# Pooling the first batch's keys on TensorE instead of VectorE, with the opening loads reordered

## The chip, the cores and the metric

The kernel runs on one core of a Trainium2 chip. The metric is the device time of one execution in microseconds; for the kernel before it is 1462.22 us, the median of 3 runs (1461.35 to 1463.22).

## The reference

Attention over pooled keys and values, then two feed-forward blocks, all in float32:

```python
B, H, S, D = 8, 8, 576, 64
k_p = k.reshape(B, H, S // 8, 8, D).mean(axis=3)      # 72 pooled keys per head
v_p = v.reshape(B, H, S // 8, 8, D).mean(axis=3)
attn = softmax(q @ k_p.T / sqrt(D))                   # per head
x = (attn @ v_p), heads side by side                  # 4608 tokens x 512
h = max(x @ w1, x @ w2, x @ w3)                       # 512 -> 768
x2 = h @ w_mid                                        # 768 -> 512
u = x2 @ w_in                                         # 512 -> 2048
out = (u - tanh(u)) @ w_out                           # 2048 -> 512
```

## The kernel before, in words

Every engine walks the same hand-made list `ORDER` (made by `make_order`, L91) and picks the entries that concern it; semaphores do the rest. Tokens are treated in 36 steps of 128 for the attention and in 9 tiles of 512 for the feed-forward blocks; the first tile's first layer is done in two halves of 256 tokens. The products of the feed-forward blocks are made as three passes over a high part and a low part of both operands, so each weight block ("piece") is loaded raw, rounded to its high part by ScalarE (`piece_high`, entry `high`) and has the remainder taken by VectorE or GpSimd (`piece_low`, entry `low`; the pieces named in `LOW_ON_POOL`, from the third weight block on, go to GpSimd). The matmuls of the attention are plain float32, and each of them appears in the profile as two instructions on PE and two weight loads on PEld.

The opening, where the change lies, runs as follows before it.

- SyncE issues all loads from one queue, in program order (L370 to L389): the four head pairs' keys of batch 0 (`k_first`, dims on partitions, 576 tokens x 4 pairs), the first 128 tokens' `q`, then, after a wait for the first keys, the second `q`, batch 0's values (`v_first`, tokens on partitions, 5 blocks of up to 128 tokens), then weight blocks, `q` and later keys and values alternately.
- TensorE multiplies a tile of ones with itself 14 times (`keep_warm`, L565), into a bank that nobody reads. VectorE meanwhile sums batch 0's keys by eights (`reduce_k`, L779), one instruction per pair, into `k_pooled`.
- TensorE makes the scores of steps 0 and 1 (`score`, L487; waits for `q` and for all four sums), pools the values by a product with a 0/1 matrix (`poolers`, `pool_first_v`, L506), does 14 more products of ones, and then `attend(0)` (L527), which waits for both steps' probabilities. VectorE takes row maxima, shifts, normalizes and transposes (L796 to L820); ScalarE does the exponentials (L661) between.
- The result goes through ScalarE (L666) and VectorE (L826) as high and low parts into `x`, and the first layer (`layer1`, L544) starts: blocks m = 0 to 5, each 3 x 12 matmuls into PSUM banks 0 to 3 in turn. ScalarE copies the first of the three banks (L672), VectorE takes the maxima of the other two (L836, L841), ScalarE and VectorE make the high and low part of `h1` (L680, L847). A bank is free for the next block once it is so read.
- After block 0 of the first half come the scores of steps 2 and 3, and in ScalarE's list their exponentials stand ahead of the high part of the fourth weight block, `("high", 3)`. GpSimd takes that block's low part (L468), for which `layer1` of block 3 waits.

```python
    o = [("kred", 0, p) for p in range(PAIRS)] + [
        ("warm", 14), ("score", 0), ("score", 1), ("pool_v",), ("warm", 14), ("norm", 0), ("high", 0), ("norm", 1),
        ("high", 1), ("low", 0), ("attend", 0), ("low", 1), ("high", 2)]
```

Of the kernel before, what the change touches and what calls it, by code (L numbers as in the profile page):

```python
# [5 lines left out]
F32 = mybir.dt.float32  # L6
F32R = mybir.dt.float32r
U8 = mybir.dt.uint8
ALU = mybir.AluOpType
# [3 lines left out]
P = 128  # L13
# [76 lines left out]

def make_order():  # L91

    o = [("kred", 0, p) for p in range(PAIRS)] + [
        ("warm", 14), ("score", 0), ("score", 1), ("pool_v",), ("warm", 14), ("norm", 0), ("high", 0), ("norm", 1),
        ("high", 1), ("low", 0), ("attend", 0), ("low", 1), ("high", 2)]
    waiting = []

    def then(*entries):
        for e in entries:
            o.append(e)  # L100
            if e[0] == "score" and e[1] in LAST_STEP[:-2]:
# [12 lines left out]
    def split(*pieces):  # L114
        return [(part, i) for i in pieces for part in ("high", "low")]

    waiting.extend([[("kred", 1, 0), ("kred", 1, 1)], [("kred", 1, 2), ("kred", 1, 3)],
                    [("vred", 1, 0)], [("vred", 1, 1)], [("vred", 1, 2)]])
    after_l1 = [[("score", 2), ("score", 3), ("high", 3), ("norm", 2)], [("high", 4), ("norm", 3)], [("high", 5)],
                [("high", 6)], [("attend", 1)], [("high", 7)]]  # L120
    for m in range(MC1):
        l1(0, m, 0, HALF)
        then(*after_l1[m])
        if m > 1:
            fill()

    for t in range(NT):
        a = 4 * t + 4
        after_l1 = [[("score", a), ("score", a + 1), ("norm", a)], [("norm", a + 1)], [],
                    [("score", a + 2), ("score", a + 3), ("norm", a + 2)], [("norm", a + 3)], []]  # L130
        after_l2 = [[], [("attend", t + 2)], [], []]
        if t == 0:
            after_l2 = [[], [], [("attend", t + 2)], []]
        if t == 0:
            after_l1[4:] = [[], [("norm", a + 3)]]
        if t == NT - 1:
            after_l1 = [[("load", ("out", 0)), ("load", ("in", 0)), ("load_x2",)],
                        split(8) + [("load", ("out", 1)), ("load", ("in", 1)), ("x2split",)],
                        split(9, 10) + [("load", ("out", 2)), ("load", ("in", 2))],
                        split(11, 12) + [("load", ("in", 3))],  # L140
                        split(13) + [("load", ("in", 4))],
                        split(14) + [("load", ("in", 5))]]
# [27 lines left out]
assert [e[1] for e in ORDER if e[0] == "high"] == list(range(len(PIECES) - len(LATE)))  # L170


def fused_attention_mlps(nc, q, k, v_0, v, w123_in, w_mid, w_in, w_out, out):
    x2_dram = nc.dram_tensor("x2_scratch", (KC1, P, TOKENS), F32, kind="Internal").ap()

    with ExitStack() as ctx:
        def sem(name):
            return ctx.enter_context(nc.semaphore(name))
# [10 lines left out]
        def overlay(*lists):  # L189
# [39 lines left out]
        (_, w_mid_raw, k_first, v_first), (q_t, k_raw, v_raw, k_pooled, v_pooled, probs, row_max, row_sum,  # L229
         row_eps, row_inv, _, w_mid_s, h1, first_copy, best, x2_stage), (w_out_raw,), (  # L230
            w_out_s, u_sq, poly, tanh_h, g, is_big) = overlay(
            front + [("w_mid_raw", mid_shape, F32), ("k_first", [P, PAIRS, KEYS, POOL], F32), ("v_first", [P, 5, DM], F32)],
            attention + [("w_mid_s", mid_shape, F32R), ("h1", h1_shape, F32R)] + work,
            [("w_out_raw", [P, MC2, 2, DM], F32)],
            [("w_out_s", [P, MC2, 2, DM], F32R), ("u_sq", [P, 2, TB], F32),
# [13 lines left out]
        shift_ready = sem("shift_ready")  # L249
        ones_ready = sem("ones_ready")  # L250
        q_in = [sem(f"q_in{n}") for n in range(QSLOTS)]
        k_first_in = [sem(f"k_first_in{n}") for n in range(PAIRS)]
        v_first_in = [sem(f"v_first_in{n}") for n in range(2)]
        poolers_made = sem("poolers_made")
        v_first_summed = sem("v_first_summed")
# [78 lines left out]
        def _(sp):  # L334
# [7 lines left out]
            def load_k(b, p):  # L342
                if b >= B:
                    return
                i = PAIRS * (b - 1) + p
                if i >= 2:
                    sp.wait_ge(k_reduced, PAIRS + i - 1)
                sp.dma_start(k_raw[:, i % 2].rearrange("p n t -> p (n t)"), k[b, p]).then_inc(k_in[i % 2], 16)

            def load_v(b, p):  # L350
                if b >= B:
# [15 lines left out]
                sp.dma_start(x2_raw[(t + 1) % 2][:, 1], x2_dram[:, :, bass.ds(t * TB, TB)].rearrange("c p n -> p c n"))\  # L367
                    .then_inc(x2_in, 16)

            for p in range(PAIRS):  # L370
                sp.dma_start(k_first[:, p].rearrange("p n t -> p (n t)"), k[0, p]).then_inc(k_first_in[p], 16)
            load_q(0)
            sp.wait_ge(k_first_in[0], 16)
            load_q(1)
            sp.dma_start(v_first[:, 0:4], v_0[0:4 * P].rearrange("(u p) f -> p u f", p=P)).then_inc(v_first_in[0], 16)
            sp.dma_start(v_first[0:D, 4], v_0[4 * P:S]).then_inc(v_first_in[1], 16)
            load_piece(0)
            load_q(2)
            load_piece(1)
            load_q(3)  # L380
            load_piece(2)
            for p in range(2):
                load_k(1, p)
            load_piece(3)
            load_piece(4)
            for p in range(2):
                load_v(1, p)
# [84 lines left out]
        def _(pe):  # L472
# [2 lines left out]

            def score(n):
                pe.wait_ge(q_in[n % QSLOTS], 16 * (n // QSLOTS) + 16)
                pe.wait_ge(k_reduced, PAIRS * ((n * P + P - 1) // S) + PAIRS)
                if n >= 2:
                    pe.wait_ge(shifted, n - 1)  # L480
                    wait_x(pe, product_of(n) - 1)
                for g in range(GROUPS):
                    b = (n * P + g * BLK) // S
                    for pr in range(PAIRS):
                        for odd in range(2):
                            half = slice(odd * D, (odd + 1) * D)
                            mm = pe.matmul(scores_of(n)[pr * BLK:(pr + 1) * BLK, odd, g, :],  # L487
                                           q_t[half, n % QSLOTS, pr, g * BLK:(g + 1) * BLK],
                                           k_pooled[half, b % 2, pr, :], start=True, stop=True)
                mm.then_inc(scored, 1)  # L490

            def open_bank(entry, n=0):
# [2 lines left out]
                    pe.wait_ge(drained[bank], before)  # L495
                return bank

            def pool_first_v():

                pe.wait_ge(poolers_made, 3)  # L500
# [67 lines left out]
            for entry in ORDER:  # L568
                if entry[0] == "warm":
                    keep_warm(entry[1])  # L570
                if entry[0] == "pool_v":
                    pool_first_v()
                if entry[0] == "score":
# [73 lines left out]
        def _(act):  # L647
            def piece_high(i):
                act.wait_ge(piece_in[i], 16)
                _, raw, hi, _ = piece(i)  # L650
                nc.scalar.activation(hi, raw, ACT.Copy).then_inc(piece_hi, 1)

            def copy_first_v():
                act.wait_ge(v_first_summed, 1)
                nc.scalar.activation(v_pooled[:, 0].rearrange("p c o d -> p (c o d)"), psum[:, 3, 0:3 * P], ACT.Copy)\
                    .then_inc(v_first_pooled, 1)
# [42 lines left out]
            for entry in ORDER:  # L699
                if entry[0] == "high":  # L700
                    piece_high(entry[1])
                if entry[0] == "pool_v":
                    copy_first_v()
                if entry[0] == "score":
# [62 lines left out]
        @block.vector  # L767
        def _(dve):
            def reduce_k(b, p):
                if b == 0:  # L770
                    dve.wait_ge(k_first_in[p], 16)
                    src = k_first[:, p]
                else:
                    i = PAIRS * (b - 1) + p
                    dve.wait_ge(k_in[i % 2], 16 * (i // 2) + 16)
                    if b >= 2:
                        dve.wait_ge(scored, LAST_STEP[b - 2] + 1)
                    src = k_raw[:, i % 2]
                nc.vector.tensor_reduce(k_pooled[:, b % 2, p, :], src, AX.X, ALU.add).then_inc(k_reduced, 1)  # L779

            def reduce_v(b, p):
                i = 3 * (b - 1) + p
# [192 lines left out]
```

## Time and profile before

| | |
|---|---|
| median of 3 runs | 1462.22 us |
| the profiled execution | 1461.79 us |
| its span | 1459.9 us |
| PE busy | 1448.3 us (99% of the span) |
| PEld busy (weight loads) | 1198.4 us (82%) |
| DVE / ACT / POOL busy | 903.5 / 506.0 / 25.7 us |

The sum of an edit is made against the profiled execution, 1461.79 us; the median of the runs lies 0.43 us above it. PE is busy in all but about 11.6 us of the span. Times in the rows are microseconds from the span's start.

### The profile page before, as it was taken

To read this page: it belongs to the slowest core of one execution; us is meant where nothing else is said; L and a number is where in the kernel's file an instruction comes from. 1 tells how busy PE (TensorE), PEld (TensorE's weight loads), DVE (VectorE), ACT (ScalarE), POOL (GpSimd) and SP (SyncE) were. 2 spreads that over 40 slices of the span, in tenths; PEclk is the share of its full clock that TensorE was granted. 3 is DMA by queue.
4 is the path that set the end of the run, shared out by engine and by line. 5 is a ranking of instruction groups with operands and counts; after the bars stand their busy time and mean duration, and the time that the engine had idled before them with its cause. 6 is when DMAs were issued, how large, how long until landed. Compare 5 with 4: busy or idle time off the path is not lost.

```text
span 1459.9 us, 23041 instructions
## 1 busy us (share of the span) xinstructions
PE 1448.3 (99%) x9480; PEld 1198.4 (82%) x9480; DVE 903.5 (62%) x1461; ACT 506.0 (35%) x889; POOL 25.7 (2%) x28
## 2 busy tenths in 40 slices
PE   8999999999999999999999999999999999999998
PEld 7988888888888878788888888888888888888887
DVE  6856363646464626265766776667677676767666
ACT  3322122212121212144444444434444443444443
POOL 2400000000000000000000000000000000000000
PEclk9999999999999999999999999999999999999999
DMA  9241213130302000243010010100001010000000
GB/s 341 78 134 47 89 46 89 46 91 29 116 19 75 16 30 1 97 139 110 1 38 22 0 59 1 59 0 29 29 0 58 0 46 12 23 35 1 29 1 29
DMA packets 34652, 75.33 MB, mean 52 GB/s; under 512 B 3136, under 2 KB 3136, under 8 KB 34560
## 3 DMA queue, kind: packets, MB, share of 16 engines
q1 hardware_dynamic: 34560, 74.07, 15.5%
q8 instruction: 62, 1.02, 0.3%
q14 instruction: 30, 0.25, 0.1%
HBM read 55.18 MB, written 18.87 MB: 51 GB/s over the span
## 4 chain that ended last, share of the span: by engine, by line
PE 96%; DVE 2%; DMA 1%; ACT 0%; issue 0%; SPq 0%; DVEq 0%; ACTq 0%
PE psum L544 30%; PE psum L610 26%; PE psum L593 26%; PE psum L558 10%; PE psum L527 2%; PE psum L487 2%; DMA v_first<-in_v 1%; PE psum L565 0%; DVE g L884 0%; DVE poly L895 0%; DVE poly L899 0%; DVE psum L901 0%; DMA k_first<-in_k 0%; DVE probs L815 0%; DVE poly L905 0%
## 5 line engine op out<-in xcount | busy, mean ns | idle before, releaser
L544 PE MATMUL psum<-x,w 128*128 128x512 f32 (+1 forms) x2160 | 451.2, 369 | 1.7 <-DVE x L826 1.0
L544 PEld LDWEIGHTS psum<-x,w 128*128 128x128 f32 x2160 | 375.6, 188 | 71.8 <-issue 1.9
L610 PE MATMUL psum<-w_out_s,g 128*128 128x512 f32 x1728 | 415.1, 389 | 0.9 <-DVE g L884 0.9
L610 PEld LDWEIGHTS psum<-w_out_s,g 128*128 128x128 f32 x1728 | 324.3, 188 | 68.9 <-DVE g L884 1.7
L895 DVE SCALAR_TENSOR_TENSOR poly<-poly,u_sq 128x512 f32<-128x512 f32 x144 | 99.7, 692 | 235.7 <-ACT poly L734 235.7
L726 ACT ACTIVATE u_sq<-psum 128x512 f32<-128x512 f32 x144 | 86.2, 599 | 425.8 <-PE psum L593 425.8
L593 PE MATMUL psum<-x_odd,w_in_s 128*128 128x512 f32 x960 | 230.0, 389 | 0.0
L593 PEld LDWEIGHTS psum<-x_odd,w_in_s 128*128 128x128 f32 x960 | 180.2, 188 | 37.4
L593 PE MATMUL psum<-x_even,w_in_s 128*128 128x512 f32 x768 | 184.5, 389 | 0.0
L593 PEld LDWEIGHTS psum<-x_even,w_in_s 128*128 128x128 f32 x768 | 144.2, 188 | 29.9
L558 PE MATMUL psum<-h,w_mid_s 128*128 128x512 f32 x648 | 150.8, 391 | 0.0
L558 PEld LDWEIGHTS psum<-h,w_mid_s 128*128 128x128 f32 x648 | 121.0, 188 | 28.3 <-issue 3.4
L680 ACT ACTIVATE h<-best 128x512 fp32r<-128x512 f32 (+1 forms) x60 | 35.3, 589 | 275.5 <-DVE best L841 275.5
L734 ACT ACTIVATE poly<-u_sq,shift_col 128x512 f32<-128x512 f32 x144 | 104.3, 725 | 2.2 <-DVE g L884 2.2
L905 DVE COPY_PREDICATED poly<-is_big,psum 128x512 f32<-128x512 uint8 x144 | 104.9, 729 | 0.1
L884 DVE TENSOR_TENSOR g<-poly,g 128x512 fp32r<-128x512 f32 x144 | 99.7, 692 | 6.3 <-ACT g L720 1.5
L901 DVE TENSOR_TENSOR psum<-psum,tanh_h 128x512 f32<-128x512 f32 x144 | 99.8, 693 | 0.0
L899 DVE SCALAR_TENSOR_TENSOR poly<-poly,psum 128x512 f32<-128x512 f32 x144 | 98.0, 680 | 0.0
L841 DVE TENSOR_TENSOR best<-psum,best 128x512 f32<-128x512 f32 (+1 forms) x60 | 38.3, 638 | 89.2 <-PE psum L544 87.7
L720 ACT ACTIVATE g<-poly 128x512 fp32r<-128x512 f32 x144 | 90.9, 631 | 5.0 <-DVE poly L905 5.0
L727 ACT ACTIVATE tanh_h<-psum 128x512 f32<-128x512 f32 x144 | 85.5, 594 | 0.0
L836 DVE TENSOR_TENSOR best<-psum,first_copy 128x512 f32<-128x512 f32 (+1 forms) x60 | 37.5, 625 | 77.4 <-PE psum L544 77.4
(53 smaller groups left out, 697.9 us busy)
## 6 DMA issues: line engine op xcount, KB each, us to landing
v_raw<-in_v SPq DMA_DIRECT2D x21, 512.0 KB, 4.3
q_t<-in_q SPq DMA_DIRECT2D x36, 256.0 KB, 3.4
x_scratch<-x_stage SPq DMA_DIRECT2D x36, 256.0 KB, 3.1
out<-out_stage SPq DMA_DIRECT2D x36, 256.0 KB, 2.1
k_raw<-in_k SPq DMA_DIRECT2D x28, 288.0 KB, 2.9
x_raw_odd<-x_scratch SPq DMA_DIRECT2D x5, 1024.0 KB, 5.2
w_raw<-in_w SPq DMA_DIRECT2D x6, 768.0 KB, 13.9
x_raw_even<-x_scratch SPq DMA_DIRECT2D x4, 1024.0 KB, 5.1
```

The lines of the kernel that those rows point to most:

```text
L544: mm = pe.matmul(psum[:, bank, 0:hi - lo], w123[:, m, ws, n, c, :], x[:, xs, c, lo:hi], start=(c == 0 and ws + xs == 0), stop=(c == KC1 - ...
L558: mm = pe.matmul(psum[:, bank, :], w_mid_s[:, ws, m, c * P:(c + 1) * P], h1[:, xs, m, :], start=(m == 0 and ws + xs == 0), stop=(m == MC1 ...
L593: mm = pe.matmul(psum[:, 4 + m % 4, :], w_in_s[:, m, ws, c, :], xs_tile[:, xs, c, :], start=(c == 0 and ws + xs == 0), stop=(c == KC1 - 1 ...
L610: mm = pe.matmul(psum[:, j, :], g[:, m % 4, gs, j * P:(j + 1) * P], w_out_s[:, m, ws, :], start=(m == 0 and gs + ws == 0), stop=(m == MC2 ...
L720: nc.scalar.activation(g[:, m % 4, 0, :], poly[:, m % 2], ACT.Copy).then_inc(g_hi_ready, 1)
L726: nc.scalar.activation(u_sq[:, m % 2], bank, ACT.Square).then_inc(sq_done, 1)
L734: nc.scalar.activation(poly[:, m % 2], u_sq[:, m % 2], ACT.Square, bias=shift_col[:, 0:1])\
L884: nc.vector.tensor_tensor(g[:, m % 4, 1, :], poly[:, m % 2], as_f32(g[:, m % 4, 0, :]), ALU.subtract).then_inc(g_ready, 1)
L895: nc.vector.scalar_tensor_tensor(out=p, in0=p, scalar=OFFSET, in1=u, op0=ALU.add, op1=ALU.mult)\
L899: nc.vector.scalar_tensor_tensor(out=p, in0=p, scalar=C2, in1=bank, op0=ALU.mult, op1=ALU.mult)
L901: nc.vector.tensor_tensor(bank, bank, tanh_h[:, m % 2], ALU.subtract).then_inc(dve_step, 1)
L905: nc.vector.copy_predicated(p, is_big[:, m % 2], bank).then_inc(h_drained, 1)
```

## The change

Batch 0's keys arrive as tokens on partitions (a new input `k_0`, 576 rows of 512 floats) in five loads, four of 128 tokens and one of 64. TensorE pools them: per block of tokens four products, each with 128 dims of the keys as the weights and 16 columns of `poolers` as the moving operand (8 columns for the last block), into bank 1; ScalarE copies the 128 x 288 result into `k_pooled`, and `score(0)` waits for that copy. The products of ones are dealt out between the blocks: 8, 2, 2 and 1 ahead of the scores, 8 before the values' pooling, 10 after it. VectorE's four sums for batch 0 go away. SyncE no longer waits before the second `q`, and the second weight block is loaded ahead of the third `q`, the fourth ahead of batch 1's first keys. `("high", 3)` moves ahead of the scores of steps 2 and 3.

```diff
-    o = [("kred", 0, p) for p in range(PAIRS)] + [
-        ("warm", 14), ("score", 0), ("score", 1), ("pool_v",), ("warm", 14), ("norm", 0), ("high", 0), ("norm", 1),
-        ("high", 1), ("low", 0), ("attend", 0), ("low", 1), ("high", 2)]
+    o = [("warm", 8), ("pool_k", 0), ("warm", 2), ("pool_k", 1), ("warm", 2), ("pool_k", 2), ("warm", 1), ("pool_k", 3),
+         ("pool_k", 4), ("score", 0), ("score", 1), ("warm", 8), ("pool_v",), ("warm", 10), ("norm", 0), ("high", 0),
+         ("norm", 1), ("high", 1), ("low", 0), ("attend", 0), ("low", 1), ("high", 2)]
...
-    after_l1 = [[("score", 2), ("score", 3), ("high", 3), ("norm", 2)], [("high", 4), ("norm", 3)], [("high", 5)],
+    after_l1 = [[("high", 3), ("score", 2), ("score", 3), ("norm", 2)], [("high", 4), ("norm", 3)], [("high", 5)],
...
-                sp.dma_start(k_raw[:, i % 2].rearrange("p n t -> p (n t)"), k[b, p]).then_inc(k_in[i % 2], 16)
+                sp.dma_start(k_raw[:, i % 2].rearrange("p n t -> p (n t)"), k[b - 1, p]).then_inc(k_in[i % 2], 16)
...
-            for p in range(PAIRS):
-                sp.dma_start(k_first[:, p].rearrange("p n t -> p (n t)"), k[0, p]).then_inc(k_first_in[p], 16)
+            for u in range(5):
+                rows = min(P, S - u * P)
+                sp.dma_start(k_first[0:rows, u], k_0[u * P:u * P + rows]).then_inc(k_first_in[u], 16)
             load_q(0)
-            sp.wait_ge(k_first_in[0], 16)
             load_q(1)
...
             load_piece(0)
+            load_piece(1)
             load_q(2)
-            load_piece(1)
+            load_piece(2)
             load_q(3)
-            load_piece(2)
+            load_piece(3)
             for p in range(2):
                 load_k(1, p)
-            load_piece(3)
             load_piece(4)
...
             def score(n):
                 pe.wait_ge(q_in[n % QSLOTS], 16 * (n // QSLOTS) + 16)
-                pe.wait_ge(k_reduced, PAIRS * ((n * P + P - 1) // S) + PAIRS)
+                if n == 0:
+                    pe.wait_ge(k_first_pooled, 1)
+                if n * P + P > S:
+                    pe.wait_ge(k_reduced, PAIRS * ((n * P + P - 1) // S))
...
+            def pool_first_k(u):
+
+                rows, keys = slice(0, P if u < 4 else D), P // POOL if u < 4 else D // POOL
+                if u == 0:
+                    pe.wait_ge(poolers_made, 3)
+                pe.wait_ge(k_first_in[u], 16)
+                for pr in range(PAIRS):
+                    at = pr * KEYS + u * P // POOL
+                    mm = pe.matmul(psum[:, 1, at:at + keys], k_first[rows, u, pr * P:(pr + 1) * P],
+                                   poolers[rows, 0, 0:keys], start=True, stop=True)
+                if u == 4:
+                    mm.then_inc(k_first_summed, 1)
...
+            def copy_first_k():
+                act.wait_ge(k_first_summed, 1)
+                nc.scalar.activation(k_pooled[:, 0].rearrange("p a n -> p (a n)"), psum[:, 1, 0:PAIRS * KEYS], ACT.Copy)\
+                    .then_inc(k_first_pooled, 1)
...
+                if entry == ("pool_k", 4):
+                    copy_first_k()
```

The first place where instructions move is the head of TensorE's program. There `ones` are the products of ones, `k_pooled,q_t` the scores, `v_first,poolers` the values' pooling, `turned,v_pooled` `attend(0)`, `x,w` the first layer. Before:

```order
L565 MATMUL psum<-ones 128x128 x14
L487 MATMUL psum<-k_pooled,q_t 32x72 x64
L506 MATMUL psum<-v_first,poolers 32x128 x20
L565 MATMUL psum<-ones 128x128 x14
L527 MATMUL psum<-turned,v_pooled 64x256 x24
L544 MATMUL psum<-x,w 128x256 x36
```

and with the change, where `poolers,k_first` is the new pooling of the keys:

```order
L582 MATMUL psum<-ones 128x128 x8
L511 MATMUL psum<-poolers,k_first 128x16 x4
L582 MATMUL psum<-ones 128x128 x2
L511 MATMUL psum<-poolers,k_first 128x16 x4
L582 MATMUL psum<-ones 128x128 x2
L511 MATMUL psum<-poolers,k_first 128x16 x4
L582 MATMUL psum<-ones 128x128
L511 MATMUL psum<-poolers,k_first 128x16 x4
L511 MATMUL psum<-poolers,k_first 128x8 x4
L492 MATMUL psum<-k_pooled,q_t 32x72 x64
L582 MATMUL psum<-ones 128x128 x8
L523 MATMUL psum<-v_first,poolers 32x128 x20
```

Twenty matmuls on whole 128-column weights now stand ahead of the scores, and 13 products of ones in place of 14.

The second place is ScalarE after the first layer's block 0; `w<-w_raw` is a weight block's high part, `probs` the exponentials. Before:

```order
L666 ACTIVATE x<-psum 128x256 x4
L651 ACTIVATE w<-w_raw 128x1536
L672 ACTIVATE first_copy<-psum 128x256
L680 ACTIVATE h<-best 128x256
L661 ACTIVATE probs<-probs 128x8x72 x2
L651 ACTIVATE w<-w_raw 128x1536
L672 ACTIVATE first_copy<-psum 128x256
```

and with the change:

```order
L690 ACTIVATE x<-psum 128x256 x4
L670 ACTIVATE w<-w_raw 128x1536
L696 ACTIVATE first_copy<-psum 128x256
L704 ACTIVATE h<-best 128x256
L670 ACTIVATE w<-w_raw 128x1536
L685 ACTIVATE probs<-probs 128x8x72 x2
L696 ACTIVATE first_copy<-psum 128x256
```

The high part of the fourth block has moved ahead of both exponentials.

## Rows read from the trace of the kernel before

**Rows 1.** The page, busy time by engine and the costliest group.

```profile
PE 1448.3 (99%) x9480; PEld 1198.4 (82%) x9480; DVE 903.5 (62%) x1461; ACT 506.0 (35%) x889; POOL 25.7 (2%) x28
```

**Rows 2.** Chain that ended last, opening: start, us, what.

```profile
0.81 2.92 DMA k_first<-in_k
...
4.60 8.20 DMA v_first<-in_v
12.93 1.95 PE psum L506 x40
14.88 4.35 PE psum L565 x28
```

**Rows 3.** Timeline, DVE: start, us, engine, line, op, names, shapes, [idle before <-releaser].

```profile
6.83 1.48 DVE L779 TENSOR_REDUCE k_pooled<-k_first 128x72 f32<-128x576 f32 x2 [1.45 <-DMA k_first<-in_k]
9.37 0.76 DVE L796 TENSOR_REDUCE row_max<-psum 128x8 f32<-128x576 f32 x1 [1.06 <-PE psum L487]
...
17.19 0.98 DVE L820 STREAM_TRANSPOSE turned<-probs 128x768 f32<-128x768 f32 x1
```

**Rows 4.** Timeline, TensorE, its matmuls and weight loads.

```profile
8.43 1.39 PEld L487 LDWEIGHTS psum<-k_pooled,q_t 64*32 64x32 f32 x128 [1.45 <-DMA q_t<-in_q]
8.46 1.54 PE L487 MATMUL psum<-k_pooled,q_t 64*32 64x72 f32 x128 [1.28 <-DVE k_pooled L779]
...
19.16 1.55 PE L527 MATMUL psum<-turned,v_pooled 32*64 32x256 f32 x48
...
27.89 8.89 PE L544 MATMUL psum<-x,w 128*128 128x256 f32 x72
```

**Rows 5.** Windows, PE: stretch, its length, PE busy (matmuls), granted clock, DMA share, GB/s.

```profile
1.00:6.50 5.50, 5.40 (x25) 1.00 0.81 235
...
10.00:12.80 2.80, 0.00 (x0) 1.00 1.06 320
...
14.80:16.90 2.10, 2.10 (x14) 0.50 1.02 406
17.10:19.10 2.00, 2.00 (x19) 1.00 1.00 399
```

**Rows 6.** Line L565, 2 to 6 us, then 17.5 to 19 us: durations min/median/max in ns.

```profile
L565 PEld LDWEIGHTS psum<-ones x21: 333/333/334, 1.7 to 6.0; 128*128 128x128 f32 x21
...
L565 PEld LDWEIGHTS psum<-ones x14: 192/192/193, 17.4 to 18.8; 128*128 128x128 f32 x14
```

**Rows 7.** Line L565 in 5 to 7.3 us, and line L487 in 8 to 11 us: durations.

```profile
L565 PE MATMUL psum<-ones x12: 274/421/422, 4.7 to 6.9; 128*128 128x128 f32 x12
...
L487 PEld LDWEIGHTS psum<-k_pooled,q_t x128: 102/106/108, 8.4 to 9.7; 64*32 64x32 f32 x128
```

**Rows 8.** Timeline, ScalarE.

```profile
14.94 0.49 ACT L655 ACTIVATE v_pooled<-psum 128x384 f32<-128x384 f32 x1 [1.85 <-PE psum L506]
...
18.51 1.48 ACT L651 ACTIVATE w<-w_raw 128x1536 fp32r<-128x1536 f32 x1 [1.07 <-DMA w_raw<-in_w]
...
33.23 0.36 ACT L672 ACTIVATE first_copy<-psum 128x256 f32<-128x256 f32 x1
```

**Rows 9.** Timeline, 32 to 41 us: DVE, POOL and TensorE around block 3.

```profile
32.38 0.76 DVE L815 TENSOR_TENSOR probs<-probs,row_inv 128x576 f32<-128x576 f32 x1
33.41 8.23 POOL L468 TENSOR_TENSOR w<-w_raw,w 128x512 fp32r<-128x512 f32 x6 [5.51 <-ACT w L651]
35.47 0.77 DVE L847 TENSOR_TENSOR h<-best,h 128x256 fp32r<-128x256 f32 x1 [0.48 <-ACT h L680]
...
37.67 1.56 DVE L815 TENSOR_TENSOR probs<-probs,row_inv 128x576 f32<-128x576 f32 x1
...
40.17 0.39 DVE L836 TENSOR_TENSOR best<-psum,first_copy 128x256 f32<-128x256 f32 x1
40.61 5.80 PEld L544 LDWEIGHTS psum<-x,w 128*128 128x128 f32 x48 [0.25 <-DVE best L836]
```

**Rows 10.** Waits: PE on the fourth weight block, one wait.

```profile
PE psum L544 <- POOL w L468: 0.6, 1, 0.6
```

More of the change, by code:

```diff
@@ L170, with fused_attention_mlps @@
 assert [e[1] for e in ORDER if e[0] == "high"] == list(range(len(PIECES) - len(LATE)))
-def fused_attention_mlps(nc, q, k, v_0, v, w123_in, w_mid, w_in, w_out, out):
+def fused_attention_mlps(nc, q, k_0, v_0, k, v, w123_in, w_mid, w_in, w_out, out):
     x2_dram = nc.dram_tensor("x2_scratch", (KC1, P, TOKENS), F32, kind="Internal").ap()
@@ L231, in fused_attention_mlps @@
             w_out_s, u_sq, poly, tanh_h, g, is_big) = overlay(
-            front + [("w_mid_raw", mid_shape, F32), ("k_first", [P, PAIRS, KEYS, POOL], F32), ("v_first", [P, 5, DM], F32)],
+            front + [("w_mid_raw", mid_shape, F32), ("k_first", [P, 5, DM], F32), ("v_first", [P, 5, DM], F32)],
             attention + [("w_mid_s", mid_shape, F32R), ("h1", h1_shape, F32R)] + work,
@@ L251, in fused_attention_mlps @@
         q_in = [sem(f"q_in{n}") for n in range(QSLOTS)]
-        k_first_in = [sem(f"k_first_in{n}") for n in range(PAIRS)]
+        k_first_in = [sem(f"k_first_in{n}") for n in range(5)]
+        k_first_summed = sem("k_first_summed")
+        k_first_pooled = sem("k_first_pooled")
         v_first_in = [sem(f"v_first_in{n}") for n in range(2)]
@@ L346, in load_k @@
                 if i >= 2:
-                    sp.wait_ge(k_reduced, PAIRS + i - 1)
-                sp.dma_start(k_raw[:, i % 2].rearrange("p n t -> p (n t)"), k[b, p]).then_inc(k_in[i % 2], 16)
+                    sp.wait_ge(k_reduced, i - 1)
+                sp.dma_start(k_raw[:, i % 2].rearrange("p n t -> p (n t)"), k[b - 1, p]).then_inc(k_in[i % 2], 16)
             def load_v(b, p):
@@ L496, in open_bank @@
                 return bank
+            def pool_first_k(u):
[9 more added lines that the diff above has]
+                    mm.then_inc(k_first_summed, 1)
             def pool_first_v():
-                pe.wait_ge(poolers_made, 3)
                 for n in range(2):
@@ L570, in _ @@
                     keep_warm(entry[1])
+                if entry[0] == "pool_k":
+                    pool_first_k(entry[1])
                 if entry[0] == "pool_v":
@@ L769, in reduce_k @@
             def reduce_k(b, p):
[L770 to L779, printed above, removed]
+                i = PAIRS * (b - 1) + p
+                dve.wait_ge(k_in[i % 2], 16 * (i // 2) + 16)
+                if b >= 2:
+                    dve.wait_ge(scored, LAST_STEP[b - 2] + 1)
+                nc.vector.tensor_reduce(k_pooled[:, b % 2, p, :], k_raw[:, i % 2], AX.X, ALU.add).then_inc(k_reduced, 1)
             def reduce_v(b, p):
@@ L950 @@
               .transpose(2, 0, 1, 3).reshape(STEPS, P, PAIRS * P),
-        "k": k.reshape(B, PAIRS, 2, S, D).transpose(0, 1, 2, 4, 3).reshape(B, PAIRS, P, S),
+        "k_0": k[0].transpose(1, 0, 2).reshape(S, DM),
         "v_0": v[0].transpose(1, 0, 2).reshape(S, DM),
+        "k": k[1:].reshape(B - 1, PAIRS, 2, S, D).transpose(0, 1, 2, 4, 3).reshape(B - 1, PAIRS, P, S),
         "v": np.pad(v[1:].reshape(B - 1, PAIRS, 2, KEYS, POOL, D), ((0, 0),) * 3 + ((0, KPAD - KEYS), (0, 0), (0, 0)))
```

## The prediction

> **What bounds the kernel now.** The page comes first: PE is busy for 1448.3 of 1459.9 us [rows 1], so a time can only move where PE idles or does work that nobody needs. The chain of waits shows where that is in the part that the change touches: keys' load, values' load until 12.80, the values' pooling, then 4.35 us of products of ones, then `attend(0)` [rows 2]. TensorE is in order, so whatever stands in its list ahead of `attend(0)` delays it; from that product on, the first layer follows at a fixed distance and PE is nearly dense to the end. The whole change is therefore worth what it does to the start of `attend(0)`, 19.16 [rows 4], plus what it does at the fourth weight block.
>
> Two chains lead to 19.16. VectorE's: the keys' last two sums start at 6.83 when the third load has landed and run without a further wait to 8.31, so the fourth load was there by 7.57; the first row maximum starts at 9.37 and the second transpose ends at 17.19 + 0.98 = 18.17 [rows 3]. TensorE's: scores from 8.46, idle from 10.0 to 12.9, values' pooling, 14 products of ones to 19.16. TensorE's is the later by 0.99 us. The reason is in the windows: after the idle stretch the granted clock is 0.50 for a while, and 28 instructions take 4.35 instead of about 3.4 us (28 x 0.12) [rows 2, 5]. The scores themselves waited for both: `q` released the weight load at 8.43, the last sum the matmul at 8.46 [rows 4].
>
> **The change, part by part.** I follow TensorE, since the keys' pooling is now its own.
>
> *Prices.* A product of ones is two instructions. In 1.0 to 6.5 us 25 take 5.40, 0.216 each; in 17.1 to 19.1 they are below 0.12 [rows 5]. The granted clock reads 1.00 in both, but the durations differ: weight loads of 333 ns against 192 [rows 6], and the opening's matmuls go from 421 to 274 ns only among those that start up to 6.9 [rows 7]. So the opening begins at the lower level (1.2 GHz), whatever its row says, and is at 2.4 GHz from about 6.8.
>
> *One block of keys* is 4 matmuls, 8 instructions, each with a new 128-column float32 weight and only 16 moving columns. No row shows that pair. What does a weight of 128 columns cost when the matmul beside it is short? From above: the first layer's 72 instructions with such a weight and 256 columns take 8.89 us, 0.123 each [rows 4]. From below: the scores' 128 instructions take 1.54, 0.012 each, with 32-column weights in separate parts of the array [rows 4]; four of them load 128 columns, so 0.048. Between them: a weight load lasts 192 ns for 128 columns and 106 for 32 [rows 6, 7], so 96 more columns cost 86 ns, and 128 cost 0.115. I take 0.12, the row of the same shape, hence 0.96 us a block; at the lower clock the 0.213 of the products of ones, 1.70 us. The last block has half the rows but as many weight columns; it costs the same. The Trainium skill, "TensorE: Matmul & The Clock Gate", section "LDWEIGHTS", says that the time of a weight load goes with its columns and not its rows, at columns / 1.2 ns; that is 107 ns here and would make the blocks 0.86 us and the scores about 0.4 us earlier than by the row.
>
> *The path to the scores.* Products of ones from 1.10 (after `ones`, as before): 16 x 0.216 = 3.46, to 4.56. Block 0 (landed 3.73 [rows 2]) 1.70, to 6.26. Two products 0.86 less 0.15 for the rise of the clock, to 7.0. Block 1, 0.96, to 7.95. Two products at 0.12, to 8.45. Block 2 to 9.4. One product to 9.65. Blocks 3 and 4 to 11.55. The loads are the same 1152 KB in five pieces for four, in a queue that is full, so the last block lands near 7.6 as before and is no longer what is waited for. Then ScalarE's copy of 288 columns, between 0.36 for 256 and 0.49 for 384 [rows 8], with 0.1 for the two hand-overs: the scores start at 12.05 instead of 8.46. VectorE's four sums (3.0 us) vanish, but nothing else was waiting for VectorE then; that is worth nothing.
>
> *From the scores to `attend(0)`.* VectorE's chain is unchanged, 18.17 - 8.46 = 9.71 us, so it ends at 21.76. TensorE: scores to 13.6, 8 products to 15.55, values (landed 12.80) at most 1.95, to 17.5, 10 products to 19.9. So now VectorE is the later, `attend(0)` starts at about 21.8 instead of 19.16: **+2.65 us**. The 0.99 us of unneeded products is gone and has been overpaid by 3.6 us of later scores.
>
> *The loads.* The removed wait held back the second `q` and all behind it by some tenths; but the queue moves 400 GB/s in those stretches [rows 5], so landings are set by bytes. The second weight block lands earlier by one `q`: ScalarE waited 1.07 for it and was done at 19.99 [rows 8], before `attend(0)` ended at 20.7. With everything later this slack only grows. Nothing.
>
> *The fourth weight block.* PE waits 0.6 us for GpSimd's low part before block 3 [rows 10]. With `("high", 3)` ahead of the exponentials, GpSimd starts some 5 us earlier and this wait goes. But the third group of that block needs a bank that VectorE has read: L836 starts at 40.17, and the weight loads there already idled 0.25 us for it [rows 9]. So the wait moves to VectorE and nothing is won by itself. VectorE's own time shifts with GpSimd's: the product L815 took 0.76 while GpSimd was idle and 1.56 beside it [rows 9]. GpSimd's earlier work now lies beside the first of them (+0.8 at most) and no longer beside L847 (0.77, perhaps -0.35). Bounds -0.35 to +0.5; I take 0, since the two are of opposite sign. On ScalarE the exponentials wait for VectorE's shifts anyway, so 1.47 us ahead of them delays nothing.
>
> *Sum.* 1461.79 + 2.65 = 1464.4 for an execution like the profiled one; the median of the runs was 0.43 higher, so **1464.9 us**, +0.18%. A measurement of this kernel tells from no change only what exceeds about 0.2%, 2.9 us; this forecast lies just inside it. Its own range, from the weight prices 0.107 and 0.123 and the fourth block's bounds, is 1464.0 to 1465.7.
>
> **Rivals.**
>
> *The blocks are cheap and the loads set the pace.* If short matmuls let the weights of four column groups load beside each other, as the scores' do, a block is 8 x 0.048 = 0.38 us (0.77 at the lower clock): blocks end at 5.3, 6.8, 7.65, 8.3 and 8.7, the scores start at 9.2, VectorE's chain ends at 18.9 and `attend(0)` gains 0.2: 1462.0. If a block is still cheaper, the last landing at 7.6 leads to scores at 8.5, the chain ends at 18.2 and 0.95 is gained: 1461.3. For it: the many close starts in the scores. Against it: those use separate 32-column parts, and these blocks the whole width. The same page of the Trainium skill, "Back-to-back issue gap", gives about 60 cycles (25 ns) between matmuls of 1 to 64 columns; by that alone a block would be 0.2 us, the lower end of this rival, but the table leaves weight loads out. Chance 0.27.
>
> *The clock stays low or falls.* This one ends slower. The opening reached 2.4 GHz after 5.7 us of dense products [rows 5, 7]. Now 1.7 of those are weight loads with little streaming between. If they don't count as work, everything up to the scores goes at the lower rate: 26 x 0.216 + 40 x 0.213 = 14.1 us from 1.10, scores at 15.7, `attend(0)` at 25.4, +6.3: 1468.5. A milder form: PE idles some 2 us before `attend(0)`, and after the 2.8 us of idleness before, the granted clock fell to 0.50 for over 2.1 us [rows 5]. If it falls in the first layer, or between blocks 2 and 4, for 2.1 to 3 us, half of that time is lost, 1.0 to 1.5 us: about 1466.2. It decides from a loss of 0.25 us on, where the sum passes 1465.1. The Trainium skill, same page, "Part 1: The HAM clock gate", calls the low rate the default, released by activity; it doesn't say here whether weight loads are activity, and no row shows it. Chance 0.31.
>
> *The reorder at the fourth block does what it is for.* PE's 0.6 us go: 1464.3 in place of 1464.9; inside my range.
>
> **Numbers.** Forecast 0.40, cheap blocks 0.27, clock 0.31, anything else 0.02. The forecast's range crosses 1465.1 for a third of its chance (0.13). Slower by over 0.2%: 0.13 + 0.31 + 0.01 = 0.45. Within: 0.27 + 0.25 = 0.52. Faster by over 0.2% would need 1459.3, below even the cheapest blocks: 0.03. The range 1461.2 to 1468.5 takes in both rivals' prices and leaves out their tails, nearly 2 in 10.
>
> **What would show it.** In the profile after: eight matmuls of a block in 0.96 us; scores starting near 12.0 after a ScalarE copy, released by PE and not by a load; the last key landing near 7.6; products of ones finished near 19.9 and `attend(0)` released by VectorE's transpose at 21.8; no PE wait on GpSimd before block 3, but one of 0.5 to 1.3 us on VectorE in it. Scores before 10 would show the blocks cheap; a granted clock of 0.50, or weight loads of 333 ns, between 7 and 27 us the clock rival. The forecast is wrong if `attend(0)` starts before 20.5 or after 22.7.

## The result and the profile after

The changed kernel takes 1465.47 us, the median of 14 runs (1462.79 to 1468.62), against 1461.59 us for the kernel before in its own 14 runs (1461.14 to 1463.67). The ratio is 1.0024, with a 95% interval of 1.0016 to 1.0032: slower by about a quarter of a per cent. (The ratios in this document are the ones on record with each run; they are not the quotients of the two medians, which can differ from them in the fourth digit.) The profiled execution took 1468.62 us, with a span of 1466.9 us where the one before had 1459.9. The 14 runs fall into groups, six at 1462.8 to 1463.2, three at 1465.3 to 1466.6 and five at 1468.2 to 1468.6; the profile shows one of the last.

First the chain of waits of the changed kernel, as [rows 2] for the one before: start, us, what.

```profile
1.11 3.78 PE psum L582 x16
4.89 1.52 PE psum L511 x8
6.41 1.04 PE psum L582 x4
...
12.14 3.34 PE psum L511 x16
15.50 0.42 ACT k_pooled L674
15.92 0.14 issue
16.05 1.29 PE psum L492 x63
17.44 0.77 DVE row_max L817
...
25.25 0.99 DVE turned L841
26.29 1.63 PE psum L544 x48
```

L582 is a product of ones, L511 the keys' pooling, L492 the scores, L544 `attend(0)`. No load stands in the chain any more. TensorE works without a gap from 1.11 to 15.5 on products of ones and blocks of keys, and the scores start at 16.05, where they started at 8.46 [rows 4]. `attend(0)` starts at 26.29 instead of 19.16, 7.13 us later, and the span is 7.0 us longer. The distance from `attend(0)` to the end is 1440.6 us, before 1440.7. Everything that happened to the time happened before `attend(0)`.

The rest of the difference is in the durations of single instructions. The lines L511 (4 to 16 us), L492 and L582 (18.2 to 20.5 us) of the changed kernel, min/median/max in ns:

```profile
L511 PEld LDWEIGHTS psum<-poolers,k_first x40: 285/333/334, 4.5 to 15.0; 128*128 128x128 f32 x32, 64*128 64x128 f32 x8
...
L492 PEld LDWEIGHTS psum<-k_pooled,q_t x128: 123/149/174, 16.0 to 17.9; 64*32 64x32 f32 x128
...
L582 PEld LDWEIGHTS psum<-ones x12: 286/333/333, 18.2 to 20.5; 128*128 128x128 f32 x12
```

A weight load of 128 columns lasts 333 ns, the value of the lower level (1.2 GHz) in [rows 6], from the first block of keys to the end of this stretch at 20.5 us; the scores' weight loads last 149 ns instead of 106 [rows 7]. TensorE was at the lower clock through the whole opening, until 20.9 us, when the durations fall to 192 ns. In the kernel before it was up at about 6.8.

At the fourth weight block, TensorE, GpSimd and VectorE of the changed kernel, as [rows 9]:

```profile
33.35 1.50 PE L492 MATMUL psum<-k_pooled,q_t 64*32 64x72 f32 x122
35.99 0.32 PE L492 MATMUL psum<-k_pooled,q_t 64*32 64x72 f32 x6 [1.14 <-issue]
36.24 17.53 PE L561 MATMUL psum<-x,w 128*128 128x256 f32 x144
...
35.78 3.78 POOL L470 TENSOR_TENSOR w<-w_raw,w 128x512 fp32r<-128x512 f32 x3 [0.76 <-ACT w L670]
...
47.22 0.39 DVE L857 TENSOR_TENSOR best<-psum,first_copy 128x256 f32<-128x256 f32 x1
```

GpSimd now starts that block's low part 6.89 us after the first layer's start (28.89 to 35.78) instead of 11.66 (21.75 to 33.41), and the wait of 0.65 us ahead of block 3 is gone. A new one has come: 1.14 us inside the scores of steps 2 and 3, for which the profile names no releaser. The first layer's start to `attend(1)` takes 24.81 us (28.89 to 53.70), before 24.80 (21.75 to 46.55): neither the gain nor the new wait shows. VectorE sets the pace here: the read that frees a bank for block 3's third group (L836 before, L857 after) starts 18.42 us after the first layer's start in the kernel before (40.17) and 18.33 in the changed one (47.22), whatever TensorE waited for until then.

### The profile page after: what moved, and what is told of

Its sections match the earlier page's. It is cut to its first block, busy times and chain, and to the rows that moved or that the text cites. A ratio compares the mean times of both kernels' runs of the same rounds, so it can differ in the third digit from the quotient of the medians.

```text
span 1466.9 us, 23129 instructions
## 1 busy us (share of the span) xinstructions
PE 1457.6 (99%) x9526; PEld 1208.3 (82%) x9526; DVE 899.8 (61%) x1457; ACT 505.9 (34%) x890; POOL 25.7 (2%) x28
## 4 chain that ended last, share of the span: by engine, by line
PE 97%; DVE 2%; ACT 0%; issue 0%; POOL 0%; DVEq 0%; ACTq 0%; POOLq 0%
PE psum L561 31%; PE psum L629 26%; PE psum L612 26%; PE psum L575 10%; PE psum L492 2%; PE psum L544 2%; PE psum L511 1%; PE psum L582 0%; DVE g L905 0%; DVE poly L916 0%; DVE poly L920 0%; DVE psum L922 0%; DVE poly L926 0%; ACT poly L760 0%; DVE turned L841 0%
## 5 line engine op out<-in xcount | busy, mean ns | idle before, releaser
L857 DVE TENSOR_TENSOR best<-psum,first_copy 128x512 f32<-128x512 f32 (+1 forms) x60 | 37.5, 624 | 75.9 <-PE psum L561 75.9
```

## The experiments

Each was timed beside the kernel before on the same chip, in 9 to 12 runs (a3 and a4 below are one run each). Theory A: the loss is the pooling matmuls ahead of the scores and the low clock that goes with them. Theory B: it comes with the loads' order, or lies behind `attend(0)`. Theory C, formed after the first four runs, says that the waits with no releaser are TensorE waiting for its next instructions to be brought from memory.

**The change without its pooling** (e2).

```diff
-    after_l1 = [[("score", 2), ("score", 3), ("high", 3), ("norm", 2)], [("high", 4), ("norm", 3)], [("high", 5)],
+    after_l1 = [[("high", 3), ("score", 2), ("score", 3), ("norm", 2)], [("high", 4), ("norm", 3)], [("high", 5)],
...
-            sp.wait_ge(k_first_in[0], 16)
...
             load_piece(0)
+            load_piece(1)
             load_q(2)
-            load_piece(1)
+            load_piece(2)
             load_q(3)
-            load_piece(2)
+            load_piece(3)
```

> The kernel before with everything of the change except the pooling of the keys: no wait ahead of the second q, second weight block ahead of the third q, fourth ahead of batch 1's keys, high part of the fourth block ahead of the scores of steps 2 and 3. Theory A (the loss is the twenty pooling matmuls ahead of the scores, and the clock they keep low): 1461.6 us as before, within 0.5; attend(0) at 19.1 to 19.2. Theory B (the loss comes with the loads or with the fourth block's order): 1463.5 to 1466, with a later landing or a longer wait in the first 45 us.

Measured: 1462.71 us against 1462.15, ratio 0.9999 (0.9990 to 1.0008). TensorE's waits of that kernel:

```profile
PE psum L505 <- DMA v_first<-in_v: 3.0, 1, 3.0
...
PE psum L543 <- DVE best L835: 0.7, 1, 0.7
```

The wait for GpSimd is gone and one of 0.7 us for VectorE stands in its place, within the same block. Theory B falls for the median. One part of the expectation missed: `attend(0)` started at 20.60 in this trace and not at 19.1, with the same instructions ahead of it, because the clock was low for longer (the values' pooling took 2.52 us instead of 1.95, the 28 products behind it 5.34 instead of 4.42). The span followed, 1461.3 us, 1440.7 after `attend(0)`.

**Each pooling matmul in four quarters** (e3).

```diff
-                    mm = pe.matmul(psum[:, 1, at:at + keys], k_first[rows, u, pr * P:(pr + 1) * P],
-                                   poolers[rows, 0, 0:keys], start=True, stop=True)
+                    for g in range(GROUPS):
+                        mm = pe.matmul(psum[g * BLK:(g + 1) * BLK, 1, at:at + keys],
+                                       k_first[rows, u, pr * P + g * BLK:pr * P + (g + 1) * BLK],
+                                       poolers[rows, 0, 0:keys], start=True, stop=True)
```

> The changed kernel with each pooling matmul cut into four on 32 weight columns each (own column group, own 32 output partitions), the same result. Theory A1 (cost is the load of 128 weight columns through the whole width): loads of four column groups run beside each other as the scores' do, a block takes 0.4 us at the full clock and about 0.8 at the lower one in place of 0.96 and 1.7, scores start at 9 to 12 in place of 12 to 16, time 1461.5 to 1464, about 2 us under the changed kernel in like clock conditions. Theory B (the loss is elsewhere): 1463 to 1468.5 as the changed kernel.

Measured: 1466.12 us against 1462.15, ratio 1.0025 (1.0015 to 1.0035). TensorE's timeline:

```profile
6.02 0.45 PE L512 MATMUL psum<-poolers,k_first 128*32 128x16 f32 x32
...
7.83 0.81 PE L512 MATMUL psum<-poolers,k_first 128*32 128x16 f32 x64
9.27 0.62 PE L492 MATMUL psum<-k_pooled,q_t 64*32 64x72 f32 x36 [0.63 <-ACT k_pooled L676]
13.66 1.70 PE L492 MATMUL psum<-k_pooled,q_t 64*32 64x72 f32 x92 [3.76 <-issue]
```

The price was right and the time, expected at 1461.5 to 1464, was not. A block takes 0.45 us at the full clock, though it has four times the instructions, and the scores start at 9.27 us: what a whole-width block costs is the load of its weights. Then TensorE stands for 3.76 us in the midst of the first step's scores, with their `q` and keys already in use, and gives the gain back.

The opening shows one thing more. Its first 16 instructions on ones are those of the changed kernel, but with quarters behind them the clock rises. The next group of products (L584, 5.4 to 5.8 us):

```profile
L584 PEld LDWEIGHTS psum<-ones x4: 186/190/192, 5.4 to 5.7; 128*128 128x128 f32 x4
```

In e11 below, with the same opening, the durations are those of the higher clock from 6.2 us on.

**Fourteen products first, then the blocks back to back** (e4).

```diff
-    o = [("warm", 8), ("pool_k", 0), ("warm", 2), ("pool_k", 1), ("warm", 2), ("pool_k", 2), ("warm", 1), ("pool_k", 3),
+    o = [("warm", 14), ("pool_k", 0), ("pool_k", 1), ("pool_k", 2), ("pool_k", 3),
```

> The changed kernel with 14 products of ones first and then the five blocks of keys back to back (no products between them). Theory A2 (the clock rises by dense streaming, and blocks of keys with short matmuls do not bring it up): the clock is up by about 7 us as in the kernel before, blocks take 0.96 us, scores start at about 12.4, attend(0) at 22.2, 1464.6 us with a small spread. If the clock rises just as late whatever is issued (its own phase): scores at 12 to 15.5 and a spread over 1463 to 1468 as in the changed kernel. Theory B: as the changed kernel, 1465.5.

Measured: 1466.03 us against 1462.15, ratio 1.0020 (1.0011 to 1.0029). Windows of TensorE: stretch, its length, busy (matmuls), granted clock, DMA share, GB/s:

```profile
6.40:8.80 2.40, 2.40 (x25) 1.00 0.94 302
8.90:12.70 3.80, 3.80 (x19) 0.50 1.07 336
12.80:13.30 0.50, 0.00 (x0) 0.50 1.09 389
```

The line L511 in the first and in the second of these stretches:

```profile
L511 PEld LDWEIGHTS psum<-poolers,k_first x20: 192/192/192, 6.5 to 8.6; 128*128 128x128 f32 x20
...
L511 PEld LDWEIGHTS psum<-poolers,k_first x17: 285/333/334, 8.8 to 12.4; 128*128 128x128 f32 x9, 64*128 64x128 f32 x8
```

The clock was up before the first block, as theory A has it, but it did not stay: after some 2.5 us of whole-width blocks, with TensorE busy all the time, the granted clock is 0.50. While it was up, the 20 weight loads of the first row started 0.112 us apart (6.50 to 8.62). The scores started at 13.37, a us later than expected, and the time missed 1464.6 by 1.4. Nor was the spread small: five runs lie at 1463.6 to 1464.4, five at 1466.0 to 1466.4 and one at 1467.7, and the trace is one of the second group.

**The opening's products with 16 columns instead of 128** (e9).

```diff
                 for _ in range(n):
-                    pe.matmul(psum[:, 0, 0:P], ones[:], ones[:], start=True, stop=True)
+                    cols = 16 if warmed[0] == 0 else P
+                    pe.matmul(psum[:, 0, 0:cols], ones[:], ones[:, 0:cols], start=True, stop=True)
+                warmed[0] += 1
```

> The kernel before with the first 14 products of ones streaming 16 columns instead of 128 (same weights, same number of weight loads; nobody reads the product). Theory A2 (weight loads with little streaming do not bring the clock up): products still take about 0.213 each instruction, weight loads last 333 ns through the values' pooling and most of the second products, which end at 20 to 21 instead of 19.16, +1 to +2 us. If weight loads count as work: clock up at about 6.8 as before, 1461.6 within 0.5.

Measured: 1462.44 us against 1462.15, ratio 1.0000 (0.9991 to 1.0009). The products of ones in the opening and the values' pooling:

```profile
L566 PEld LDWEIGHTS psum<-ones x28: 286/333/333, 1.1 to 6.8; 128*128 128x128 f32 x28
...
L506 PEld LDWEIGHTS psum<-v_first,poolers x40: 125/177/177, 12.7 to 14.7; 128*32 128x32 f32 x32, 64*32 64x32 f32 x8
```

The 28 instructions take 6.15 us, about as before (28 x 0.216 = 6.05 [rows 5]): at the lower clock 16 columns cost what 128 do, as the weight load sets the pace. And the clock, at the same TensorE busy time, no longer rises at 6.8: the scores take 2.21 us instead of 1.54, and the loads are still slow in the values' pooling. This is theory A's second half shown by itself: weight loads with little streaming did not bring the clock up here. It is one trace, but the runs agree with it: the kernel before shows a fall of the granted clock inside its span in 30 of the 31 runs beside these (mean 0.996 to 0.999), e9 in none of its 11 (mean 1.000), and a fall needs a rise before it. The Trainium skill, "TensorE: Matmul & The Clock Gate", "Part 1: The HAM clock gate", says that activity releases the clock. In these rows TensorE was busy for 6.15 us, nearly all of it with weight loads, and the clock was not released. The expected loss of 1 to 2 us was not there: `attend(0)` came at 19.66, 0.5 us later, since before the change the clock is low around the values' pooling too.

**The changed kernel again** (a2, a3, a4): no edit.

> The changed kernel once more, unaltered, for a profile in which the clock may rise at another moment. Theory A (the time is set by when the clock rises): if this execution's weight loads fall to about 192 ns earlier than at 20.7 us, attend(0) starts earlier by as much as the blocks, products and scores then save; fully at 2.4 GHz from 7 us on, a block takes 0.9 to 1.0 us, scores start near 12 and the span is 1462 to 1463. The distance from attend(0) to the end stays that of the kernel before within 0.3 us. Theory B (something behind attend(0) also costs): that distance is longer by over 1 us.

> The changed kernel once more, one look, for an execution in which the clock rises earlier than in the two profiles so far (both at about 20.5 us). Theory A: the start of attend(0) and the span move together, with a distance from attend(0) to the end of the span as in the kernel before (1440.7) within 0.3 us; with the clock up at 7 us, scores start near 12 and attend(0) near 21.8.

> As a3_after_again: another look at the same kernel, since the moment at which the clock rises differs between executions.

Measured: 1465.73 us against 1462.37, ratio 1.0022 (1.0013 to 1.0031), the 12 runs again in groups (five at 1463.6 to 1464.1, three at 1465.6 to 1465.9, four at 1468.6 to 1468.7). The two single runs (a3, a4) took 1468.98 and 1468.38 us. All three traces show the late rise once more, at 19.7 to 20.1 us, and `attend(0)` at 26.28 or 26.29, with 1440.4 to 1441.0 us behind it. None showed an earlier rise, so what the faster groups' openings look like is not shown. The mean granted clock of each run's span says something of them. It is 1.000 in all nine runs at 1468.2 to 1468.7 us (five of the first set, four of this one), 0.999 in the eleven at 1462.8 to 1464.1 and 0.995 to 0.997 in the six between. A mean under 1 means that the clock fell inside the span, and so had risen before; in the traces with the late rise it never falls again. The faster runs therefore had a rise and a fall that the slowest lack, which fits an earlier rise; when it came is not on record.

**Quarters, with the loads held back** (e11): e3 and one line.

```diff
             load_q(1)
+            sp.wait_ge(scored, 1)
             sp.dma_start(v_first[:, 0:4], v_0[0:4 * P].rearrange("(u p) f -> p u f", p=P)).then_inc(v_first_in[0], 16)
```

> The kernel e3 (pooling in 32-column quarters) with one wait more: SyncE issues the values' load and all behind it only once the first scores are made. In e3 TensorE idled 3.76 us inside the scores with no releaser, from 9.9 to 13.7, while the one 16 KB transfer of the instruction queue ran at 11.3. Theory C (TensorE waited for its next instructions, behind a full load queue): the stall inside the scores goes or falls under 1.5 us, scores end near 11, attend(0) at 19 to 20 in a like clock, 1462 to 1463.5. Rival (the stall is the wait for the second q, or tied to the number of instructions alone): the stall stays at 3 to 4 us, and the time rises above 1466.

Measured: 1466.35 us against 1462.37, ratio 1.0025 (1.0016 to 1.0034). TensorE's timeline; then the DMA queue that the profile names `instruction`, in 7.6 to 7.8 us of this kernel and in 10.9 to 11.1 us of e3 (packets, MB, share of the DMA engines):

```profile
9.62 0.62 PE L493 MATMUL psum<-k_pooled,q_t 64*32 64x72 f32 x36 [0.63 <-ACT k_pooled L677]
10.45 1.17 PE L493 MATMUL psum<-k_pooled,q_t 64*32 64x72 f32 x92 [0.20 <-issue]
11.54 2.05 PE L585 MATMUL psum<-ones 128*128 128x128 f32 x16
17.47 2.52 PE L526 MATMUL psum<-v_first,poolers 128*32 128x128 f32 x40 [3.87 <-DMA v_first<-in_v]
```

```profile
q8 instruction: 1, 0.02, 40.8%
...
q8 instruction: 1, 0.02, 39.2%
```

The stop is at the same instruction, after 36 of the 128, but lasts 0.20 us instead of 3.76. The instruction queue's transfer of 16 KB runs from 7.68 to 8.99 us here; in e3, behind a full load queue, from 10.97 to 12.22. TensorE goes on 1.46 us after the transfer's end here (10.45) and 1.44 us after it in e3 (13.66). That is theory C: TensorE had run out of instructions, and the loads ahead of them made the stop long. The time did not improve and came out as the rival had it: the values now come late (3.87 us of waiting), and the first layer's two waits are as in e3.

**The kernel before with its products dealt out** (e5, e6, e12, e13).

```diff
-        ("warm", 14), ("score", 0), ("score", 1), ("pool_v",), ("warm", 14), ("norm", 0), ("high", 0), ("norm", 1),
+        ("warm", 14), ("score", 0), ("score", 1), ("warm", 11), ("pool_v",), ("warm", 16), ("norm", 0), ("high", 0), ("norm", 1),
```

That is e5 and, with e2's edits, e6. e12 has 14, 11 and 9 products at these three places; e13 has 12, 8 and 12, made so:

```diff
-                for _ in range(n):
-                    pe.matmul(psum[:, 0, 0:P], ones[:], ones[:], start=True, stop=True)
+                for _ in range(n // 4):
+                    pe.matmul(psum[:, 0, :].rearrange("p (a n) -> p a n", a=4), ones[:],
+                              ones[:].unsqueeze(1).to_broadcast([P, 4, P]), start=True, stop=True)
```

> The kernel before with its 14 products ahead of attend(0) dealt out as 11 ahead of the values' pooling and 16 behind it, so that TensorE does not idle from 10.0 to 12.9. Theory A: the clock is kept, the values' pooling and the 16 products go at the full rate, TensorE is ready at 17.9 and VectorE's transpose releases attend(0) at 18.2: 0.5 to 1.0 us faster than before, 1461.2. Rival: the clock falls anyway or rises late in some executions, and 13 more products at the lower rate delay the values' pooling past 12.9: 1462.5 to 1465.

> e5 together with the loads' order and the fourth block's order of the change (a candidate to beat both): theory A gives the time of e5 within 0.4, since e2 showed the two orders to be worth nothing.

> The kernel before with 11 products ahead of the values' pooling and 9 behind it (e5 has 16). In e5 the 16 products ended 1.3 us after VectorE's transpose, because TensorE stood 0.6 us for its next instructions within them. Theory A with theory C (products and instruction supply set TensorE's arrival): TensorE is ready at 17.5 to 18.3, the transpose releases attend(0) at 18.2 to 18.4, 0.5 to 1.0 us under e5's trace and 1461.0 to 1461.4. Rival (nothing left to win, VectorE or the later stretch takes it back): 1461.9 as e5.

> The kernel before with each four products of ones made as one of 512 moving columns (same streaming, a quarter of the instructions), 12 ahead of the scores, 8 ahead of the values' pooling, 12 behind it in the old count. Theory C: no stall without a releaser on TensorE in the first 35 us; theory A: attend(0) released by VectorE at about 18.3, 1460.8 to 1461.4. Rival: as e5, 1461.9.

| kernel | us | before beside it | ratio (95%) | `attend(0)` | span |
|---|---|---|---|---|---|
| e5 | 1461.88 | 1462.37 | 0.9995 (0.9987 to 1.0004) | 19.52 | 1459.8 |
| e6 | 1461.88 | 1462.37 | 0.9994 (0.9985 to 1.0003) | 19.29 | 1460.2 |
| e12 | 1460.19 | 1461.73 | 0.9993 (0.9984 to 1.0002) | 17.82 | 1458.3 |
| e13 | 1460.88 | 1461.73 | 0.9991 (0.9982 to 1.0000) | 18.56 | 1459.6 |

TensorE's timeline of e12:

```profile
9.53 2.72 PE L565 MATMUL psum<-ones 128*128 128x128 f32 x22
12.76 1.43 PE L506 MATMUL psum<-v_first,poolers 128*32 128x128 f32 x40 [0.50 <-DMA v_first<-in_v]
14.12 0.71 PE L565 MATMUL psum<-ones 128*128 128x128 f32 x4
15.97 1.83 PE L565 MATMUL psum<-ones 128*128 128x128 f32 x14 [1.14 <-issue]
17.82 1.56 PE L527 MATMUL psum<-turned,v_pooled 32*64 32x256 f32 x48
```

The products stream in the gap in which TensorE idled, the granted clock no longer falls behind it, the values' pooling takes 1.43 us instead of 1.95, and TensorE reaches `attend(0)` at the moment at which VectorE's transpose ends (16.79 + 0.98 = 17.77). Of the 1.34 us by which `attend(0)` is earlier, 0.39 come from the scores, which started at 8.07 in this trace for 8.46. In e5 TensorE was 1.3 us too late for it, as its 16 products came on top of a stop of 0.59 us. e5 missed its forecast of 1461.2 by 0.7, and e12's 1460.19 lies 0.8 under its own. The mechanism is shown by the traces; in the times all four intervals reach 1, so no gain over the kernel before is established. e12's and e13's medians lie 1.5 and 0.9 us under it. e13 had no stop without a releaser up to 50 us, as theory C has it, but another wait of 1.80 us, for the second `q`. Against the changed kernel, each of the four is faster by its own comparison with the kernel before (0.9995 or less, where the changed kernel has 1.0016 or more).

## Why the prediction was right, and where it was not

The number held: 1464.9 was forecast and 1465.47 measured, +0.24% where the text gave +0.18%, with 0.45 for slower by over 0.2% and 0.52 for within it. The way there was only in part the forecast's, and by its own sign of being wrong it failed: `attend(0)` was to start between 20.5 and 22.7 us and starts at 26.28 or 26.29 in all four traces.

That the number held is in good part luck. The loss was forecast as 2.65 us and is 3.9 us between the two medians (1465.47 - 1461.59); the forecast started from 1462.22, 0.63 us above the later median of the kernel before, and this hid half of the miss. And the median falls between groups of runs: only two of the 14 lie in the forecast's own range of 1464.0 to 1465.7.

**Only the start of `attend(0)` counts: right.** In the kernel before, in all four traces of the changed one and in e2, e4, e5, e6, e9 and e12, 1440.3 to 1441.0 us lie between it and the end; e13 has 1441.1, e11 1441.3 and e3 1443.0. The last two have a stop of 2.1 us in the first layer, and e3 besides a granted clock of 0.50 from 36.1 to 39.4 us.

**A block's price: right.** At the full clock 0.112 us an instruction (e4) for 0.12, at the lower one 8 in 1.71 us (a block and two products recur every 2.56 us, of which 0.85 are the products) for 1.70. The estimate from the Trainium skill, "TensorE: Matmul & The Clock Gate", section "LDWEIGHTS", 0.107, was a little too low, as 0.12 was a little too high. The cheap rival fell: whole-width blocks never came near its 0.38 us, and only e3's quarters, each in its own column group, load their weights beside each other (0.45 us a block). The Trainium skill, same page, "Back-to-back issue gap", has 25 ns between matmuls of so few columns; with a new whole-width weight for each, e4 has 112.

**The clock at full rate from 6.8 us: the step that failed,** in every profiled execution. "Two products 0.86 less 0.15 for the rise of the clock" is where it stands in the working; no rise came before 19.7 us in any of the four traces (20.9 in the first). What happened is the second rival's full form, which had 0.31: scores at 15.7 and 1468.5 us were worked out there, 16.05 and 1468.62 measured. The cause named there, weight loads with little streaming between, is borne out by e9, in which they left the clock low, and by e4, in which a clock that was up fell while TensorE did nothing else. In e3, with quarters in their place, the clock rose at 5.4 us. The rival missed one term: the scores themselves are slower at the lower clock (2.21 us instead of 1.54), so VectorE's chain took 10.2 us from their start and not 9.71. Scores 4.0 us later than 12.05 and a chain 0.47 us longer are the whole 4.5 us between the forecast's 21.8 and 26.29. The median of the runs lies between this case and the forecast's, and the groups at 1463 and 1465 us would be earlier rises; the granted clocks under a2 fit that reading, and no trace shows it.

**VectorE as the new releaser of `attend(0)`: right,** at 26.23 in place of 21.76. **The copy** took 0.41 us, as bounded.

**The loads and the fourth block at nothing: right** (e2, 0.9999). In e2 the wait moved from GpSimd to VectorE as said (0.74 us), and the first layer's start to `attend(1)` stayed 24.75 us for 24.80. In the changed kernel the wait on VectorE did not appear, since the stop of 1.14 us ahead of it had let VectorE catch up.

**Not foreseen:** the stops for want of instructions. In the changed kernel they cost nothing (0.28 us in the values' pooling and 1.14 in the scores of steps 2 and 3, both under VectorE's chain), but in e3 one of 3.76 us took back what the cheaper blocks had won.

## What to carry to other kernels

A matmul with few moving columns on a full-width float32 weight costs its weight load, and in e4 and e9 it did not keep TensorE's clock up or bring it there. Cut into column groups it was half as dear (0.45 us a block for 0.9), though four times the instructions brought TensorE sooner to the stop for want of more. Don't count such instructions among those that fill a gap. Before moving work onto an engine ahead of a chain, set its whole duration at the lower clock against the engine that does it now for nothing; here VectorE's four sums, hidden behind the loads, were replaced by 40 instructions in front of everything. By the traces of e5 and e12, filler products belong into the gap in which TensorE would idle, and as few after it as the next releaser allows; in the times no gain is established.

## What the runs showed of the hardware that was not expected

- The granted clock reads 1.00 from the start of a trace until its first change, also while TensorE runs at the lower level: durations of 421 ns for a product and 333 ns for a weight load are the evidence, 275 and 192 ns at the full clock.
- TensorE stops with no releaser after its 222nd matmul instruction in six kernels of this case: in the changed kernel (12 into the values' pooling), in e3 and e11 (36 into the scores), in e5, e6 and e12 (4 into the second products). Each time it goes on 1.4 to 1.5 us after a 16 KB transfer of the instruction queue has ended: at 22.40 us after 20.93 in the changed kernel, 13.66 after 12.22 in e3, 10.45 after 8.99 in e11, 15.97 after 14.55 in e12. In the kernel before the transfer has ended at 14.52, TensorE gets there at 18.7 and doesn't stop. A second stop of this kind comes 253 or 254 matmul instructions later in the changed kernel, e4, e5, e6 and e12. Only e11 against e3 shows what lengthens a stop: loads ahead of that transfer. What starts the transfer is not shown.
